# Attention in front of two MLP stages: gate rows on 96 partitions, exponents of four heads in one matmul, their rows brought by DMA, and a new order within a unit

## What is computed

```
m_new  = max(f[t] + m, i[t])
f_stab = exp(f[t] + m - m_new);  i_stab = exp(i[t] - m_new);  m = m_new
C = f_stab * C + i_stab * outer(v[t], k[t]);   n = f_stab * n + i_stab * k[t]
y[t] = sigmoid(o[t]) * (C @ q[t]) / max(|n . q[t]|, 1)
```

## Time and profile before

| | |
|---|---|
| median of 3 runs | 1013.81 us (1010.05 to 1015.14) |
| the profiled execution | 1013.65 us, its span 1011.9 us |
| PE busy | 984.6 us, 97% of the span |
| DVE, ACT, POOL busy | 434.4, 306.0, 83.4 us |
| mean granted TensorE clock | 0.991 |

### The profile page before, as it was taken

How to read it: one execution, slowest core, us unless ns; L and a number is a source line. 1 busy time by engine, 2 the same in 40 slices (tenths; PEclk the granted TensorE clock), 3 DMA queues, 4 the chain that set the end, 5 groups by cost and what they waited for, 6 DMA issues and landing times.

```text
span 1011.9 us, 15246 instructions
## 1 busy us (share of the span) xinstructions
PE 984.6 (97%) x5489; PEld 868.8 (86%) x5500; DVE 434.4 (43%) x804; ACT 306.0 (30%) x568; POOL 83.4 (8%) x149
## 2 busy tenths in 40 slices
PE   6998899999999989999999999999999999999998
PEld 3888788888778978988999999889999998899997
DVE  8677746645553265244244223424423332442222
ACT  6556344434442221132122112312212221221111
POOL 7345200000000323000000000000000000000000
PEclk7999999999999999999999999999999999999999
DMA  9843300030030003003000300300120030000000
GB/s 134 183 70 46 92 22 1 0 115 1 1 108 8 1 1 115 1 0 114 1 0 0 115 1 0 114 0 0 44 70 0 0 114 0 0 0 1 26 26 26
DMA packets 67168, 39.19 MB, mean 39 GB/s; under 512 B 51488, under 2 KB 63264, under 8 KB 67136
## 3 DMA queue, kind: packets, MB, share of 16 engines
q1 hardware_dynamic: 67136, 38.78, 16.2%
HBM read 36.81 MB, written 1.97 MB: 38 GB/s over the span
## 4 chain that ended last, share of the span: by engine, by line
PE 92%; DVE 5%; ACT 2%; issue 1%; POOL 0%; DVEq 0%; POOLq 0%; ACTq 0%
PE psA L1190 44%; PE psB L1228 11%; PE psB L1230 11%; PE psB L1229 11%; PE psB L1206 2%; PE psB L1208 2%; PE psB L1207 2%; PE psB L1097 2%; PE psA L1075 1%; PE psB L1213 1%; PE psB L1212 1%; PE psB L1085 1%; PE psA L1068 1%; DVE ug L838 1%; DVE den L835 1%
## 5 line engine op out<-in xcount | busy, mean ns | idle before, releaser
L952 DVE SCALAR_TENSOR_TENSOR gl<-psA,gh 128x512 fp32r<-128x512 f32 x192 | 132.8, 692 | 341.2 <-ACT gh L702 341.0
L702 ACT ACTIVATE gh<-psA 128x512 fp32r<-128x512 f32 x192 | 114.9, 598 | 537.4 <-PE psA L1190 537.4
L1228 PE MATMUL psB<-w2s,gh 128*128 128x320 f32 x768 | 237.6, 309 | 0.0
L1229 PE MATMUL psB<-w2s,gh 128*128 128x320 f32 x768 | 237.3, 309 | 0.0
L1230 PE MATMUL psB<-w2s,gl 128*128 128x320 f32 x768 | 237.2, 309 | 0.0
L1190 PE MATMUL psA<-xh,w1h 128*128 (+1 forms) x480 | 190.5, 397 | 0.0
L1190 PE MATMUL psA<-xl,w1h 128*128 (+1 forms) x480 | 189.8, 395 | 0.0
L1190 PE MATMUL psA<-xh,w1l 128*128 (+1 forms) x480 | 188.9, 394 | 0.0
L1229 PEld LDWEIGHTS psB<-w2s,gh 128*128 128x128 f32 x768 | 144.3, 188 | 5.5
L1228 PEld LDWEIGHTS psB<-w2s,gh 128*128 128x128 f32 x768 | 144.2, 188 | 5.1
L1230 PEld LDWEIGHTS psB<-w2s,gl 128*128 128x128 f32 x768 | 144.4, 188 | 0.0
(11 more groups left out here) (178 smaller groups left out, 939.0 us busy)
## 6 DMA issues: line engine op xcount, KB each, us to landing
raw<-in_moe_w_dram SPq DMA_DIRECT2D x16, 640.0 KB, 8.3
raw<-in_moe_w_dram SPq DMA_DIRECT2D x8, 1024.0 KB, 5.3
raw<-in_moe_w_dram SPq DMA_DIRECT2D x16, 256.0 KB, 6.1
raw<-in_moe_w_out_dram SPq DMA_DIRECT2D x4, 640.0 KB, 9.6
raw<-in_moe_w_in_dram SPq DMA_DIRECT2D x2, 1024.0 KB, 6.0
qs<-in_q_dram SPq DMA_DIRECT2D x12, 160.0 KB, 3.4
ks<-in_k_dram SPq DMA_DIRECT2D x12, 160.0 KB, 3.9
vz<-in_v_dram SPq DMA_DIRECT2D x24, 80.0 KB, 3.7
```

The lines of the kernel that those rows point to most:

```text
L702: act.activation(gh[:, f % RING, :], h_ps[:, f % HB, :], ACT.Relu).then_inc(ghi_ok, 1)
L952: dve.scalar_tensor_tensor(out=gl[:, f % RING, :], in0=h_ps[:, f % HB, :], scalar=0.0, in1=gh[:, f % RING, :].bitcast(F32), op0=ALU.max, o ...
L1228: pe.matmul(bank, gh[:, slot, cols], W2S[par][:, f, 0, :], start=first, stop=False)
L1229: pe.matmul(bank, gh[:, slot, cols], W2S[par][:, f, 1, :], start=False, stop=False)
```

## The change

- The running maximum is scanned as before, then one DMA issued by ACT spreads it over 96 partitions, one for each (batch, head, chunk); i and f are loaded in that shape too (`ci`, `cf`). All further row steps are single instructions on 96 partitions, on DVE alone.
- `exponents(n)` is one matmul for each four heads, two in all, of `lhs[b]` and `rhs[b]`. The rows that change with the unit are brought into these by four DMAs out of `parts` (`expo_rows`): one for the left side, three for the right. There is one `lhs` and one `rhs` for each batch, so the DMAs of unit n wait for the exponents of unit n-2. Two of unit 0's are issued by ACT, all the others by SP, between the loads of the units.
- The matmul masks only as far as a column 96; what is left, the last 32 queries of the table, POOL sets to zero in `ex` by `corner(n)`, for which `weigh(n)` now waits.
- Order in a unit, PE: exponents(n), inter(n-1), transposes(n), intra(n-1), y_transposes(n-2), state of n-1, scores(n). DVE: sums(n-1) (the former finish_y up to the reciprocal), new state (n-1), weigh(n), finish_y(n-1) (the last two multiplications), low parts (n-2). ACT does `high_parts` last in a unit.
- `low_piece` waits for `yy` of the unit before, pieces come in units 3 to 10, the last output gates are loaded behind six units, and the last unit's state is no longer prepared. The MLP starts with three hidden tiles inside the last unit.

```diff
+    PARTS = 3
+    AR = H * PARTS
+    M0 = AR + PARTS
+    CB = 96
+    PIECE_OF = {3 + n: n for n in range(PIECES)}
...
+        lhs = [asb(f"lhs{b}", [P, L], BF16) for b in range(B)]
+        rhs = [asb(f"rhs{b}", [P, H, L], BF16) for b in range(B)]
+        parts = asb("parts", [BH * NC, 2, PARTS, L], BF16)
...
-        def last_parts(eng, part):
-
-            c0, c1 = GATE_PARTS[part]
-            cols = slice(c0 * L, c1 * L)
-            eng.wait_ge(part_ok, 2 * part + 2)
-            eng.tensor_tensor(b_parts[ROWS[2]:ROWS[2] + BH, cols], rest2[:, 1, cols], mid[:, 1, cols], ALU.subtract)
-            eng.tensor_tensor(a_parts[ROWS[2]:ROWS[2] + BH, cols], rest2[:, 0, cols], mid[:, 0, cols],
-                              ALU.subtract).then_inc(parts_ok, 1)
...
+        def expo_rows(eng, n, sides):
+
+            c, b = n // B, n % B
+            rows = slice(b * H * NC + c, (b + 1) * H * NC, NC)
+            for k in sides:
+                if k < 0:
+                    eng.dma_start(lhs[b][0:AR, :], parts[rows, 0, :, :]).then_inc(expo_in[b], 16)
+                else:
+                    eng.dma_start(rhs[b][AR + k:AR + k + 1, :, :], parts[rows, 1, k, :]).then_inc(expo_in[b], 16)
...
+            def expo_load(n):
+
+                at_least(sp, x_done, n - B + 1)
+                expo_rows(sp, n, range(-1, PARTS))
...
+            load_qk(0)
+            sp.dma_start(cf[:], f_gate.rearrange("b h (c s) -> (b h c) s", s=L)).then_inc(chunk_in, 16)
+            sp.dma_start(ci[:], i_gate.rearrange("b h (c s) -> (b h c) s", s=L)).then_inc(chunk_in, 16)
+            load_v(0)
             load_gates_out(0)
-            for j in range(1, U_IT):
-                load_unit(0, j)
+            load_qk(1)
+            load_v(1)
+            sp.wait_ge(lhs_ok, B)
+            sp.wait_ge(rhs_ok[1], 1)
+            sp.wait_ge(parts_ok, 1)
+            expo_rows(sp, 0, (-1, PARTS - 1))
+            expo_load(1)
+            for n in range(2, U_IT):
+                load_qk(n)
+                load_v(n)
+            for n in range(2, U_IT):
+                expo_load(n)
             load_gates_out(1)
             sp.dma_start(wg_raw[:, 0:KT, :], w_gate[0:KT * P, :].rearrange("(t p) e -> p t e", p=P)).then_inc(wg_in, 16)
             sp.dma_start(wg_raw[0:DR, KT, :], w_gate[KT * P:DM, :]).then_inc(wg_in, 16)
             sp.dma_start(wg_raw[DR:P, KT, :], w_gate[KT * P:DM, :]).then_inc(wg_in, 16)
             load_stage(0, w_in[:, 0:FW], w_out[0:FW, :])
-            load_gates_out(2)
-            with sp.Fori(1, NU // U_IT) as i:
-                for j in range(U_IT):
-                    load_unit(i, j)
+            for n in range(U_IT, NU):
+                if n == 2 * U_IT - 1:
+                    load_gates_out(2)
+                load_qk(n)
+                load_v(n)
+                expo_load(n)
...
+            def corner(n):
+
+                pool.wait_ge(exp_done, n + 1)
+                late = ex[:, :, CB:L]
+                pool.affine_select(out=late, in_=late, compare_op=ALU.is_ge, fill=0.0, base=CB,
+                                   pattern=[[0, H], [1, L - CB]], channel_multiplier=-1).then_inc(corner_ok, 1)
...
+            corner(0)
             pool.wait_ge(gates_ok, 2)
-            for j in range(2, U_IT):
-                pool_unit(0, j)
-
-            pool.wait_ge(wg_in, 48)
-            pool.tensor_copy(wg[:, :, 0:E], wg_raw[:]).then_inc(wg_step, 1)
-            pool.wait_ge(wg_step, 1)
-            pool.tensor_tensor(wg[:, :, E:2 * E], wg_raw[:], wg[:, :, 0:E].bitcast(F32), ALU.subtract).then_inc(wg_step, 1)
-            with pool.Fori(1, NU // U_IT) as i:
-                for j in range(U_IT):
-                    pool_unit(i, j)
-                    low_piece(pool, 0, 0, (i - 1) * U_IT + j)
+            pool_unit(0)
+            for n in range(1, NU):
+                corner(n)
+                if n < NU - 1:
+                    pool_unit(n)
+                if n in PIECE_OF:
+                    pool.wait_ge(yy_done, n)
+                    low_piece(pool, 0, 0, PIECE_OF[n])
...
-                high_parts(i, j - 2)
                 exponentials(i, j)
                 qk_copies(i, j)
+                high_parts(i, j - 2)
...
+            act.wait_ge(row_step, M_ROW)
+            whole = m_row[:, 0:L + 1]
+            act.dma_start(cm[:], bass.AP(tensor=whole.tensor, offset=whole.offset,
+                                         ap=[whole.ap[0], [L, NC], [1, L + 1]])).then_inc(m_in, 16)
+            act.wait_ge(kt_blank, 1)
             qk_copies(0, 0)
+            act.wait_ge(rhs_ok[0], 1)
+            act.copy(rhs[1][:], rhs[0][:]).then_inc(rhs_ok[1], 1)
+            act.wait_ge(row_step, A_AND_B)
+            act.activation(rw_row[:, 0, :], ab[:, 1, :], ACT.Exp, bias=logf[:, 0:1]).then_inc(rw_exp, 1)
+            act.activation(rw_row[:, 1, :], ab[:, 0, :], ACT.Exp, bias=ab[:, 1, L - 1:L]).then_inc(rw_exp, 1)
+            act.wait_ge(parts_ok, 1)
+            act.wait_ge(rhs_ok[1], 1)
+            expo_rows(act, 0, range(PARTS - 1))
             exponentials(0, 0)
-            first_parts(1)
             exponentials(0, 1)
             qk_copies(0, 1)
-            middle_parts(1)
-            r_and_w(1)
-            for j in range(2, U_IT):
-                act_unit(0, j)
-            out_gates(1)
-            for i in range(1, NU // U_IT):
-                for j in range(U_IT):
-                    act_unit(i, j)
-                    high_piece(0, 0, (i - 1) * U_IT + j)
-                if i == 1:
+            out_gates(0)
+            for n in range(2, NU):
+                i, j = n // U_IT, n % U_IT
+                act_unit(i, j)
+                if n in PIECE_OF:
+                    high_piece(0, 0, PIECE_OF[n])
...
+            a_side, b_side = ab[:, 0, :], ab[:, 1, :]
+            dve.wait_ge(chunk_in, 32)
+            dve.wait_ge(m_in, 16)
+            link(dve.tensor_tensor(logf[:], cf[:], cm[:, 0:L], ALU.add), 2)
+            dve.tensor_tensor(a_side, ci[:], cm[:, 1:L + 1], ALU.subtract).then_inc(row_step, 1)
+            link(dve.tensor_tensor(logf[:], logf[:], cm[:, 1:L + 1], ALU.subtract), 4)
+            link(dve.tensor_tensor_scan(b_side[:, 1:L], ones[:, 1:L], logf[:, 1:L], 0.0, ALU.mult, ALU.add), 5)
+            link(dve.tensor_tensor(a_side, a_side, b_side, ALU.subtract), A_AND_B)
+            link(dve.tensor_copy(parts[:, :, 0, :], ab[:]), 7)
+            link(dve.tensor_tensor(rest[:], ab[:], parts[:, :, 0, :], ALU.subtract), 8)
+            link(dve.tensor_copy(parts[:, :, 1, :], rest[:]), ROW_END)
+            dve.tensor_tensor(parts[:, :, 2, :], rest[:], parts[:, :, 1, :], ALU.subtract).then_inc(parts_ok, 1)
...
+            def dve_unit(i, j):
+                sums(i, j - 1)
+                new_state(i, j - 1)
+                weigh(i, j)
+                finish_y(i, j - 1)
...
                 at_least(pe, exp_done, n)
+                pe.wait_ge(expo_in[b], EXPO * (c + 1))
                 for g in range(2):
-                    bank = psA[:, g, :]
-                    h0 = b * H + 4 * g
-                    pe.matmul(bank, a_parts[:, s_rows], sel_a[:, h0:h0 + 4, :].rearrange("p h t -> p (h t)"),
-                              start=True, stop=False)
-                    for h in range(4):
-                        last = pe.matmul(bank[:, h * L:(h + 1) * L], sel_b[:, h0 + h, :], b_parts[:, s_rows],
-                                         start=False, stop=h == 3)
+                    last = pe.matmul(psA[:, g, :], lhs[b][:],
+                                     rhs[b][:, 4 * g:4 * g + 4, :].rearrange("p h t -> p (h t)"), start=True, stop=True)
...
+            def pe_unit(i, j, y=True):
+                exponents(i, j)
+                inter(i, j - 1)
+                transposes(i, j)
+                intra(i, j - 1)
+                if y:
+                    y_transposes(i, j - 2)
+                new_state(i, j - 1)
+                scores(i, j)
...
 
 
             last_i = NU // U_IT
-            y_transposes(last_i, -2)
             inter(last_i, -1)
             pe.wait_ge(w_ready, PIECES)
             pe.wait_ge(exp_done, NU)
             hidden(0, 0, 0, 0, mlp=True)
-            intra_and_state(last_i, -1, state=False)
+            intra(last_i, -1)
+            y_transposes(last_i, -2)
             hidden(0, 0, 1, 1, mlp=True)
+            hidden(0, 0, 2, 2, mlp=True)
             y_transposes(last_i, -1)
-            mlp_block(0, 0, None, done=2)
+            mlp_block(0, 0, None, done=3)
 
             pe.wait_ge(xlo_done, NU)
             with pe.Fori(1, NTB) as tb:
```

More of the change, by code:

```diff
@@ L218, in build @@
         pads = sem("pads")
-        unit_in = [sem(f"unit_in{j}") for j in range(U_IT)]
+        qk_in = [sem(f"qk_in{j}") for j in range(U_IT)]
+        v_in = [sem(f"v_in{j}") for j in range(U_IT)]
         x_done = sem("x_done")
@@ L395, in _, with where @@
             pool.memset(zero1[:], 0.0).then_inc(zero_ok, 1)
-            for tile in (at_row, past_row, head_rows):
```

(68 more changed lines are left out.)

356 lines of the change are left out of this document (126 added, 230 removed).

## The result

| | before | after |
|---|---|---|
| median of 6 runs (lowest to highest), us | 1013.80 (1009.97 to 1015.14) | 1005.38 (1004.94 to 1007.21) |
| profiled execution, us | 1013.65 | 1007.05 (span 1005.3) |
| ratio, 95% interval | | 0.9932 (0.991 to 0.9953) |

The forecast was 998 us, in a range of 990 to 1006. The change brought 8.4 us, about half of the 15.7 forecast. The time lies 0.6 us inside the upper end of the range, close to the rival of the slower start.

The account below looks back on a forecast made before the run. PE is full in the MLP, so only attention can give time; its late units wait for a DVE chain that POOL slows. Minus 4.8 to unit 4, 8.5 to intra(10), 2.4 after: minus 15.7 from 1013.65, 998 us, range 990 to 1006.

Parts of the forecast that it names:

- the rival of the slower start: Start: all 15 DMAs in full (8.9), unit 4 at 50.0, or small DMAs at 4.3: 52.2; 1002 to 1004 us; 0.15.
- the term of 4.8 us for the 15 DMAs: SP's list ahead of the weights: 15 more DMAs cost 4.8, between nothing and 8.9; weights issued from 29.4.
- the term of the queue: SP's queue before unit 4: its rows wait behind the weights, so its exponents start at 45.9 instead of 41.0.
- the first wording: Start: all 15 DMAs cost their full 8.9, so unit 4 at 50.0.
- The start alone: Gates to exponents of unit 4, without the queue: 41.0, including 2 us for a fall of the clock.
- The rival of free DMAs: SP's list: the 15 DMAs cost nothing, exponents of unit 4 at 41.0, 993 us; chance 0.20.
- ACT as next in line: Before unit 4: ACT ready at 46.8 after first piece and sigmoid, covered by late exponents; without them it costs 3.
- Exponents of unit 4 to intra(10): Middle units: 2.2, seven pitches (50.4) and 0.4 for a sigmoid make 53.0 instead of 61.5, minus 8.5.
- The pitch of 7.2: Each unit: the loop scores, weigh, transposes sets 7.2 us instead of 8.44, with `ug` and `yy` behind weigh.
- POOL as bound: Each unit: corner takes 2.5 on POOL, pitch 8.0, 5.6 us of gain lost, 1003 to 1004 us; chance 0.15.
- The tail: From intra(10) to where PE runs on without a gap: 12.1 instead of 14.5, minus 2.4.

Follow-up runs that it names:

- the new list: Changed kernel with SP's list reordered, rows of unit 4 issued by ACT, and weight pieces spread over units 4 to 10: 997.54 us.
- the rows ahead: Kernel with the new list, with exponent rows of unit 6 ahead of q and k of unit 5, then rows one unit earlier: 993.78 us.
- the run with rows by ACT: Changed kernel with only the four row DMAs of unit 4 issued by ACT, the weights staying with SP: 1001.70 us.

## Why the prediction was wrong in size, and what of it held

The step that failed is the term of 4.8 us for the 15 DMAs added to SP's list: the first weight came 9.6 us later, not 4.8. The mechanism was the right one, the size was not, and the half clock behind the stop, 2.3 us, had no term at all. That the time still fell inside the range is owed to the width of the range.

- **Unit 4's exponents: 45.9 forecast, 52.19 measured; the term of the queue failed.** The prediction took 4.8 us for the 15 added DMAs, the middle between nothing and 8.9, so the first weight at 29.4. It was 34.22, 9.6 later than in the earlier trace rows. SP was through with the loads of unit 1 at the same time as before, but then stood idle for 1.7 us (11.07 to 12.80) until the parts were made, which was in no term. SP's timeline after, columns as in the earlier trace rows:

```profile
10.56 0.51 SPq L335 DMA_DIRECT2D vz<-in_v_dram  x1
12.80 0.91 SPq L286 DMA_DIRECT2D lhs<-parts  x1
```

From there the 14 row DMAs took 9.95 (12.80 to 17.23 and 23.99 to 29.51), more than the whole 8.9. The 15 others ahead of the weights took 11.5 where they took 13.7 before (10.88 to 24.62): only these 2.3 were given back by an emptier queue (DMA share 0.03 between 15 and 18). In full is the first wording of the rival of the slower start, with unit 4 at 50.0. Its second, 52.2, is the measured number, but by chance: it had small DMAs landing in 4.3, and they landed in 1.69. From the first weight to the rows it took 13.6 (34.22 to 47.86) where 12.2 was forecast, and from there to the exponents 4.33 for 4.3. So 4.8 and 1.4 make the 6.3. What held the rows behind the weights was SP's own issue of k and v (5.10 and 4.09), and not their place among data already issued: ACT's first piece, which waits for the last weight, started at 47.54, before the rows went out at 47.86. No run shows whether rows already issued can pass the weights.
- **The start alone was right, in part by errors that cancel.** It was to give 41.0 for unit 4 without the queue; with the new list it is 41.40. In the kernel after, the maximum landed at 9.46 instead of 8.0, but the rows came sooner behind the parts, so exponents of unit 0 started at 15.91 for 15.7. There PE also waited 1.8 for the rows of unit 2, and scores of unit 3 ended at 42.8: 1.4 of the delay would have stood without unit 4's rows. The rival of free DMAs had 993, which is 993.78 with the rows ahead, though in a kernel with another list. ACT as next in line was right in kind: ACT held unit 4's scores in the run with rows by ACT, behind the wait for k. In the kernel after it was ready at 52.3, where 46.8 was forecast.
- **Exponents of unit 4 to intra(10): 53.0 forecast, 55.4 measured.** No price was set on the clock after the queue's stop, though 2 us were charged for the same at the start (20 to 24 us, where it came true). From exponents of unit 4 to intra(4) at 64.11 it took 11.9, where the same steps take 9.66 in a late unit (105.19 to 107.61, and 7.24): half clock cost 2.3.
- **The pitch of 7.2 was right, its reason only in part.** The loop scores, weigh, transposes does close at 7.24 in the new order, with both of POOL's waits, with one of them or with none. But the old order with POOL's wait and the merged matmuls gives 7.30 as well, and the wait alone 7.54. With the merged matmuls either is enough, the order by taking `ug` and `yy` out of the path, POOL's wait for the reciprocal by keeping them short there; without both it is 8.30. The prediction had no term for that wait, and in the new order it needed none. The new order without the merging was tried only with both waits (7.37). The sentence that `ug` and `yy` must leave the path to shorten the pitch missed that they could also be made short.
- **POOL as bound: no.** Corner took 0.45 (mean 447 ns of 7 between 60 and 112 us) where the rival had 2.5, and POOL idled until DVE was ready.
- **The tail: 12.1 forecast, 11.7 measured.** From 107.61 to 121.16, less the third tile of 1.83 (119.33). The rest of the kernel took 0.8 longer than before, and that was in no term.

The profiled executions thus differ by 1.5 - 6.1 - 2.8 + 0.8 = -6.6, where the forecast was -4.8 - 8.5 - 2.4; the medians differ by 8.4, since the profiled execution after is 1.7 above its median.

## What to carry to other kernels

A list of DMAs has to be costed from the last moment at which its issuer waits for data, and that wait belongs in the sum: from there small DMAs cost their full issue time each, and loads that follow large ones are held by their bytes, here also when the large ones stood in another queue. After each predicted stop of PE a price for half clock belongs in the sum. When a change has a large reordering and a one-line wait in it, try the line alone on the old kernel: here it took the pitch from 8.39 to 7.54, most of the way to the 7.26 that the reordering was credited with.

## What the runs showed of the hardware

- In the kernel after, row DMAs within SBUF of 2 and 6 KB took SP 0.62 to 0.91 us each to issue, and 1.69 to land. A spread of 48 KB over 96 partitions took 4.03 beside the `og` loads, and 4.91 beside q, k and v of unit 1.
- SP's issue of one 80 KB load took 5.65 us while the 2.8 MB of weights moved on ACT's queue.
- A DVE product of 128x320 from two tensors in SBUF took 0.49 us with POOL held off, and 1.03 to 1.13 on average with POOL's work beside it.
- PE idle from 43 us on had a granted clock of 1.00 in 43:46, 0.71 in 46:49 and 0.50 in 49:52; with PE at work again from 52.19 it was back during 56:58. With `yy` ahead of inter, a stop of 3.2 us (75.58 to 78.81) was followed by 0.50 in 80:82.
